# Seven parts in a row: the order of a fast matrix product's parts and downs, and the split of one conversion

## The reference

```python
# 1: attention with top-32 scores, 2 batches x 8 heads x 576 x 64
scores = scale * q @ k.T;  keep scores >= 32nd largest;  x = softmax(scores) @ v
# 2: x is 1152 x 512
x = ((x @ w_a) * (x @ w_b)) @ w_out                     # 512 -> 1536 -> 512
# 3: four experts, w1 512 x 1024, w2 1024 x 512
p = domain_probs / (domain_probs.sum(-1) + 1e-9)
for e in range(4):
    out += p[:, e:e+1] * (np.maximum(x @ w1[e], 0) @ w2[e])
```

## Time and profile before

| | |
|---|---|
| median of 3 runs | 832.29 us (831.46 to 832.82) |
| the profiled execution | 832.34 us |
| its span, first to last instruction | 830.5 us |
| TensorE busy (matmuls) | 783.9 us, 94% |
| VectorE, ScalarE, GpSimd busy | 571.9, 436.8, 362.1 us |
| mean granted clock of TensorE | 0.977 |

### The profile page before, as it was taken

How to read it: one execution, slowest core, us unless ns; L and a number is a source line. 1 busy time by engine, 2 the same in 40 slices (tenths; PEclk the granted TensorE clock), 3 DMA queues, 4 the chain that set the end, 5 groups by cost and what they waited for, 6 DMA issues and landing times.

```text
span 830.5 us, 14209 instructions
## 1 busy us (share of the span) xinstructions
PE 783.9 (94%) x5141; PEld 687.2 (83%) x5141; DVE 571.9 (69%) x1144; ACT 436.8 (53%) x848; POOL 362.1 (44%) x325
## 2 busy tenths in 40 slices
PE   5469899999999999999999899999999999999998
PEld 3247778888888888888897798889988898989987
DVE  6999998989999999998444543573345634483333
ACT  6687768777777777776555422342133422343221
POOL 1868773545444444445335421463035521364010
PEclk9677999999999999999999999999999999999999
DMA  9450775466545484445578002310031002120101
GB/s 240 127 154 1 242 251 175 153 189 199 178 152 175 150 281 144 160 146 184 184 244 253 0 8 69 93 36 1 26 102 52 26 1 77 56 72 1 51 1 63
DMA packets 80709, 97.93 MB, mean 118 GB/s; under 512 B 32896, under 2 KB 60032, under 8 KB 80640
## 3 DMA queue, kind: packets, MB, share of 16 engines
q1 hardware_dynamic: 79584, 96.77, 36.9%
q10 hardware_dynamic: 1056, 0.26, 0.1%
HBM read 86.00 MB, written 11.01 MB: 117 GB/s over the span
## 4 chain that ended last, share of the span: by engine, by line
PE 82%; DVE 7%; ACT 4%; issue 3%; POOL 2%; DMA 1%; ACTq 0%; SPq 0%; POOLq 0%; DVEq 0%
PE ps L795 23%; PE ps L727 21%; PE ps L634 15%; PE ps L619 8%; PE ps L547 4%; PE ps L583 4%; PE ps L560 3%; DVE m L1132 2%; DVE work L1138 2%; PE ps L592 2%; DVE work L1126 1%; POOL p_sb L1355 1%; DMA wo<-wo_d 1%; DVE m L1122 1%; ACT s_sb L878 1%
## 5 line engine op out<-in xcount | busy, mean ns | idle before, releaser
L1132 DVE MAX8 m<-work 128x8 f32<-128x576 f32 x216 | 152.7, 751 | 0.0
L727 PE MATMUL ps<-x_hi,w_hi 128*128 128x256 f32 (+1 forms) x448 | 133.1, 297 | 5.2 <-ACT p_sb L983 4.8
L795 PE MATMUL ps<-w_lo,h_hi 128*128 128x512 f32 x288 | 113.7, 395 | 0.0
L795 PE MATMUL ps<-w_hi,h_hi 128*128 128x512 f32 x288 | 113.4, 394 | 0.0
L795 PE MATMUL ps<-w_hi,h_lo 128*128 128x512 f32 x288 | 113.1, 393 | 0.0
L1355 POOL TENSOR_TENSOR p_sb<-s_sb,p_sb 128x576 f32<-128x576 f32 x72 | 101.9, 1432 | 20.5 <-ACT p_sb L884 19.9
L1416 POOL TENSOR_TENSOR u_sb<-u_sb,p_sb 128x256 f32<-128x256 f32 (+1 forms) x32 | 30.6, 956 | 174.2 <-DVE u_sb L1255 174.2
L1138 DVE MATCH_REPLACE8 work<-m,work 128x576 f32<-128x576 f32 x144 | 106.3, 747 | 0.0
L727 PEld LDWEIGHTS ps<-x_hi,w_hi 128*128 128x128 f32 x448 | 84.9, 190 | 14.6 <-ACT p_sb L983 5.7
L995 ACT ACTIVATE h_hi<-u_sb 128x256 fp32r<-128x256 f32 (+1 forms) x64 | 28.5, 445 | 106.8 <-POOL u_sb L1416 81.0
L727 PE MATMUL ps<-x_raw_lo,w_hi 128*128 128x256 f32 (+1 forms) x256 | 76.2, 298 | 0.0
(11 more groups left out here) (124 smaller groups left out, 2027.9 us busy)
## 6 DMA issues: line engine op xcount, KB each, us to landing
wo<-wo_d SPq DMA_DIRECT2D x96, 512.0 KB, 4.8
w_raw<-moe_w_in SPq DMA_DIRECT2D x32, 256.0 KB, 3.3
w_raw<-moe_w_in SPq DMA_DIRECT2D x16, 512.0 KB, 4.8
wo_d<-wo SPq DMA_DIRECT2D x12, 512.0 KB, 4.5
w_raw<-moe_w_a_in SPq DMA_DIRECT2D x4, 768.0 KB, 5.4
w_raw<-moe_w_b_in SPq DMA_DIRECT2D x4, 768.0 KB, 5.3
wo_raw<-moe_w_out_in SPq DMA_DIRECT2D x12, 256.0 KB, 3.3
x_d<-x_out_sb SPq DMA_DIRECT2D x9, 256.0 KB, 3.0
```

The lines of the kernel that those rows point to most:

```text
L727: mm = nc.tensor.matmul(ps[:, bank, 0:NH[g]], w, x, start=first and c == n == 0, stop=last and c == HK - 1 and n == 2, skip_group_check=True)
L795: mm = nc.tensor.matmul(ps[:, DOWN_BANKS[j], 0:DM], h[:, f, tok], w[:, f, :], start=m == f == n == 0, stop=m == FM - 1 and f == 1 and n == 2)
L1132: nc.vector.max(m8[:, par, i, 8 * r:8 * r + 8], work[:, i, :]).then_inc(ve_top, 1)
```

## The change

TensorE: step k runs P1, P5, P6, P2, P3, P7, then all downs of step k-1 (tile by tile, both halves of a tile together), then P4. In step 0 the last `send` stands where the downs stand.

SyncE: `load_x2` is split into its two halves and each waits for the stores it needs; for the second group the first half is issued early. The loads of w1's quarter 2 are issued ahead of the last reloads of w_out.

ScalarE and VectorE: the preparation of the second token group is cut into pieces that stand between the copies of steps 2 and 3. In step 0 `w2_high`, `y_out` and `x2_out` stand later. The buffers u3 and c21 are placed elsewhere.

```diff
-            def load_x2(g):
-                sp.wait_ge(st_x2, 16 * (TILES[0] if g == 0 else NT))
-                for j in range(2):
...
+            def load_x2(g, j):
+                first = TOK[g] + j * NH[g]
+                sp.wait_ge(st_x2, 16 * -(-(first + NH[g]) // P))
...
-            for n in range(LAST + 2):
+            for n in range(LAST + 1):
                 slot_loads(n)
             sp.wait_ge(pe_a, NP)
             sp.wait_ge(pe_b, NP)
             load_w1(0, 2)
+            slot_loads(LAST + 1)
             load_w2(0, 1)
             load_w1(0, 3)
+            load_x2(1, 0)
             load_w2(0, 2)
             slot_loads(LAST + 3)
+            load_x2(1, 1)
             sp.wait_ge(pe_w, FC * NP)
             load_w2(0, 3)
-            load_x2(1)
...
-            def downs(k, first, last):
-                tiles = TILES[step(k)[1]]
-                for i in range(first, min(last, 2 * tiles)):
-                    down(k, i // tiles, i % tiles)
+            def downs(k):
+                for j in range(TILES[step(k)[1]]):
+                    for f in range(2):
+                        down(k, f, j)
+
+            def seven(k, between):
+                p1(k)
+                p5(k)
+                p6(k)
+                p2(k)
+                p3(k)
+                p7(k)
+                between(k - 1)
+                p4(k)
 
             send(NP - 2)
             h_transpose(NP - 1)
-            p1(0)
-            p5(0)
-            p6(0)
-            send(NP - 1)
-            p2(0)
-            p3(0)
-            p7(0)
+            seven(0, lambda k: send(NP - 1))
             y_transpose(NT - 1)
-            p4(0)
             for k in range(1, STEPS):
-                few = step(k - 1)[1] == 0
-                a, b, c, d, f = (1, 2, 3, 5, 7) if few else (1, 3, 5, 7, 9)
-                p1(k)
-                downs(k - 1, 0, a)
-                p5(k)
-                downs(k - 1, a, b)
-                p6(k)
-                downs(k - 1, b, c)
-                p2(k)
-                p3(k)
-                downs(k - 1, c, d)
-                p7(k)
-                downs(k - 1, d, f)
-                p4(k)
-                downs(k - 1, f, 2 * TILES[1])
+                seven(k, downs)
...
@@ step_copies on ScalarE
                 p5_out(k)
                 if q1 is not None:
                     w1_high_raws(q1)
+                if k == FM - 2:
+                    x2_high_piece(1, 0)
+                if k == FM - 1:
+                    x2_high_piece(1, 2)
                 act.wait_ge(pe_p2, k + 1)
...
                     w1_high_sums(q1)
+                if k == FM - 2:
+                    x2_high_piece(1, 1)
+                if k == FM - 1:
+                    x2_high_piece(1, 3)
...
@@ step 0 on ScalarE
             p5_out(0)
-            w2_high(0)
-            y_out(NT - 1)
...
             hidden_high(0, 0, 1, ac_h12)
-            x2_out(NT - 1)
+            w2_high(0)
+            y_out(NT - 1)
...
             hidden_high(0, 1, 0, ac_h21)
+            x2_out(NT - 1)
...
@@ the steps on VectorE
                 if k and w1_prepared(k) is not None:
                     w1_sums(w1_prepared(k))
+                if k == FM - 2:
+                    x2_sums(1, True)
                 u2(k)
...
                 hidden_low(k, 0, 1, ac_h12, ve_l12)
+                if k == FM - 2:
+                    x2_sums(1, False)
+                if k == FM - 1:
+                    x2_low_piece(1, 2)
...
-                if k == 2:
-                    x2_sums(1)
-                    for i in range(len(X2_PIECES)):
-                        x2_low_piece(1, i)
+                if k == FM - 2:
+                    x2_low_piece(1, 0)
+                    x2_low_piece(1, 1)
+                if k == FM - 1:
+                    x2_low_piece(1, 3)
```

More of the change, by code:

```diff
@@ L87, in build @@
         x2_out_sb = sb("x2_out_sb", [P, DK, P])
+        inv_at = top[0]
         inv_b = sb("inv_b", [P, DM])
@@ L182, in build @@
         late_at += 2 * W2B
-        u3_sb = at("u3_sb", [P, NH[1]], F32, late_at)
-        c21_sb = at("c21_sb", [P, NH[1]], F32, late_at + TEMP)
-        assert late_at - 2 * W2B <= w_end and late_at + 2 * TEMP <= ring_at
+        u3_sb = at("u3_sb", [P, NH[1]], F32, inv_at)
+        c21_sb = at("c21_sb", [P, NH[1]], F32, late_at)
+        assert late_at - 2 * W2B <= w_end and late_at + TEMP <= ring_at
         def w1_whole(m, i):
@@ L412, in keep_x2 @@
                 sp.dma_start(dst, x2_out_sb[:]).then_inc(st_x2, 16)
-            def load_x2(g):
-                sp.wait_ge(st_x2, 16 * (TILES[0] if g == 0 else NT))
-                for j in range(2):
[L417 to L420, removed]
+            def load_x2(g, j):
+                first = TOK[g] + j * NH[g]
+                sp.wait_ge(st_x2, 16 * -(-(first + NH[g]) // P))
+                src = x2_d.rearrange("(c p) n -> p c n", p=P)[:, :, first:first + NH[g]]
+                dst = x2_parts[g][0][:, 2 * j:2 * j + 2, :, :].rearrange("p h c n -> p (h c) n")
+                sp.dma_start(dst, src).then_inc(ld_x2[g], 16)
             def slot_loads(n):
@@ L455, in slot_loads @@
                         load_w1(0, m)
-                    load_x2(0)
-            for n in range(LAST + 2):
+                    load_x2(0, 0)
+                    load_x2(0, 1)
+            for n in range(LAST + 1):
                 slot_loads(n)
@@ L963, in x2_high_piece @@
             def x2_high_piece(g, i):
-                if i == 0:
-                    act.wait_ge(ve_t[g], 4)
+                act.wait_ge(ld_x2[g], 32)
+                if i:
+                    act.wait_ge(ve_t[g], 3 if i == 1 else 4)
                 raw, sums, hi = x2_parts[g][0:3]
@@ L1106, in _ @@
                 step_copies(k)
-                if k == 2:
-                    for i in range(len(X2_PIECES)):
-                        x2_high_piece(1, i)
         @block.vector
@@ L1203, in w1_sums, with x2_sums @@
                 add(part[6], part[1], part[5], ALU.subtract, ve_s, 4 * q + 2)
-            def x2_sums(g):
-                dve.wait_ge(ld_x2[g], 32)
+            def x2_sums(g, first):
                 part = [x2_whole(g, i) for i in range(7)]
[L1208 to L1211, removed]
+                if first:
+                    dve.wait_ge(ld_x2[g], 32)
+                    add(part[5], part[2], part[0], ALU.subtract, ve_t[g])
+                    add(part[6], part[3], part[5], ALU.subtract, ve_t[g], 1)
+                else:
+                    add(part[2], part[3], part[2], ALU.subtract, ve_t[g])
+                    add(part[4], part[1], part[6], ALU.subtract, ve_t[g], 2)
             def x2_low_piece(g, i):
                 dve.wait_ge(ac_x2[g], i + 1)
+                dve.wait_ge(ve_t[g], 4)
                 raw, sums, hi, raw_lo, sum_lo = x2_parts[g]
@@ L1293, in _ @@
                         nc.vector.tensor_tensor(pr_n[:, :, e], pr_raw[:, :, e], pr_inv[:], ALU.mult).then_inc(ve_pr, 1)
-                    x2_sums(0)
+                    x2_sums(0, True)
+                    x2_sums(0, False)
             for i in range(2):
```

## The result

The changed kernel takes 852.05 us (median of 6, 848.76 to 856.15) against 832.32 us before (831.46 to 833.05): ratio 1.024, 95% interval 1.0205 to 1.0274. The forecast was 850.0 us. The profiled execution took 848.76 us with a span of 847.0, 16.5 us over the span of before. It is the fastest of the six: what follows explains 16.5 us, the medians lie 19.7 us apart, and no profile shows the 3.3 us between.

The account below looks back on a forecast made before the run. The last stage's second product was taken as bound by TensorE's own stream. Steps 0 to 4 cost 9.65 less 5.7 us (+3.9), six later steps +13.8: 832.3 + 17.7 = 850.0 us, likeliest case 846 to 855, overall 839 to 858.

Parts of the forecast that it names:

- The six later steps: Steps 8, 9, 16, 17, 24, 25: P7 waits for u2 behind a held addition; 2.15 or 2.45 us each, +13.8 us.
- Rest: Other waits and steps (P4 for u3, P6 for c21, P3, loads, final downs): put at nothing.
- Step 0: Wait for the w_out chunk and restarts go, y_out lies bare before the transposes: net -0.5 us, bounds -0.9 and +1.2.
- Step 1: P2 waits for ScalarE's copy of P1 without downs ahead: TensorE idles 3.0 instead of 0.75 us, +2.1 us.
- Step 2: Two second-group additions stand ahead of u2, the later one held: stall 2.4 + 0.1 us; 0.8 unheld, 3.1 both held.
- Steps 3 and 4: Low pieces delay u2 in step 3 (3.05 + 0.1 us) and P1 in step 4 (2.3 + 0.1), less 5.7 lost before.
- The row at 478.21: w2_low(3) begins within the last two low pieces, which took 2.22 us unheld while GpSimd took 3.07; speaks for 2 us less.
- the unheld bound: Step 3: stall of 1.1 us if VectorE's low pieces are not held behind GpSimd's w2_low.
- VectorE isn't held: Rival: additions and pieces beside w2_low run unheld; +1.1 us, 833.4 us, no change that shows; chance 0.08.
- the clock falls as well: Rival: clock falls after the new waits, 1.6 us each; 853.2 us with two falls, 866 with all ten; chance 0.16.
- the pieces go unheld: Rival: pieces unheld in steps 2 and 3, additions held; 3.5 us less, 846.5 us; chance 0.15.
- The slack that I gave P3: In w2_high steps P5's copy is done at about c + 2.4, P3 ready at 2.7: 0.3 us spare, no cost.

Follow-up runs that it names:

- pool_fill: Changed kernel with w2_low waiting for w1_sums, plus idle matmuls into an unused PSUM bank before P2 (step 1), P7 (step 3), P1 (step 4): 836.62 us, ratio 1.0057.
- old_fixed: Changed kernel with TensorE's old order, u2 ahead of w1_sums and the second group's additions, its low pieces moved: 830.88 us, ratio 0.9993 to the kernel before.

## Why the prediction was right, point by point

*The six later steps.* Forecast 13.8 us, measured 15.5, of which 1.6 are the one fall of the clock in step 8. The waits were 2.05 and 2.35 by forecast, 2.00 and 2.21 in the trace; with the restarts I had 2.15 and 2.45 a step, and the five steps without a fall took 2.15, 2.19 and three times 2.47 more. The mechanism is shown four ways: the old order put back, u2 moved, GpSimd moved, cover given back. The reading that carried it is that VectorE's and ScalarE's chain from c21 hangs on nothing that TensorE's new order changes, so its length could be copied from the earlier trace rows.

*Rest.* I put it at nothing, on the ground that a part or a down takes the same whichever kind went before. The 22 other steps from step 4 on took 1.3 us less: small, but there in 21 of the 22.

*Step 0.* Forecast -0.5, measured -1.1. I had y_transpose ahead of P4 in the new order, as before. The diff has P4 first, and y_out lies under it: an order read wrongly, 0.6 us.

*Step 1.* Forecast +2.1, measured +3.2. The wait was 3.1 us where I had 3.0. The clock fell in it (0.60), a cost that I kept for a rival; the wait of P3 that I had isn't there.

*Step 2.* Forecast +2.5, measured 0.0. I took one addition as held on the ground that the two requests came at the same time. In the profile after, VectorE was ahead by 0.07 us. *pool_fill*, with 2.25 us, shows that the mechanism was right; that the fall of the clock in step 1 had hidden it in the changed kernel is what its rows point to.

*Steps 3 and 4.* Forecast 3.15 + 2.4 - 5.7 = -0.15, measured +1.2. The waits were 3.14 and 2.16 us, where I had 3.05 and 2.3. The difference is the clock in step 3 (0.57), again the rival's term. GpSimd, which asked ahead of the second piece, went first, as the Trainium skill's rule in "SBUF — State Buffer", section "Who interferes with whom", has it; the two pieces took 5.05 us instead of 2.89. The row at 478.21 that spoke for the unheld bound can be read after all, in a view that begins behind the third piece:

```profile
478.22 0.82 DVE L1219 TENSOR_TENSOR x_sum_lo<-x_sum,x_hi 128x640 fp32r<-128x640 f32 x1
```

The two were given at the same time to 0.01 us, and VectorE went first. In step 3 of the changed kernel they lie 0.48 us apart.

So the terms that I put at 3.9 and 13.8 came out at 3.3 and, with the rest, 14.2. The wait of step 2 that failed to come (-2.5), step 0 (-0.6) and the rest (-1.3) worked against three falls of the clock (1.6 us in that of step 8): that the sum came so close is in part luck. *The rivals:* that VectorE isn't held is refuted by each trace; that the clock falls as well was right for three of the ten waits, and its price of 1.6 us is what step 8 shows; that the pieces go unheld came true in step 2 and not in step 3.

Left open: where the spread between the runs of the changed kernel (7.4 us against 1.6) comes from. The clock can be only a part of it. One fall of 3.4 us lowers the mean granted clock by 0.002; the executions of 848.76, 852.1 and 855.75 us had 0.972, 0.972 and 0.970. The slack that I gave P3 in the w2_high steps (0.3 us) held in the changed kernel, but wore out to waits of 0.24 us when u2 went ahead; steps 9, 17 and 25 then took 11.12 us each, against 10.63 before.

## What to carry to other kernels

When a kernel is bound by one engine's stream, regrouping that stream wins next to nothing in itself (here less than 0.1 us a step); it moves cover. Measure, for each wait it leaves bare, the other engines' chain from its own trigger in the old trace, and compare that with the cover that stays. An operation that is the first reader's on its queue (here u2) belongs ahead of work that only has to be done sometime, but look at what that work then meets: here it fell under GpSimd's subtractions, and with the old order the wait moved from P7 to P4.

## What the runs showed of the hardware

A VectorE subtraction or addition with both inputs in SBUF that is given after a GpSimd subtraction or addition has begun is held until that one is done. It ends 0.28 us behind it with 256 columns (2.59 instead of 0.42 us), 0.68 with 640 (2.88 instead of 0.82, *pool_fill*), 1.35 with 1280 (3.53 instead of 1.49, *old_fixed*). In the fourteen traces, from 430 us on, each one that began 0.05 us or more behind GpSimd's recorded start was held, and each one that began ahead of it, or 0.01 us behind, ran at its own pace. GpSimd's row is then the longer one: 3.03 us instead of 2.4 to 2.6 beside the 0.82 us of VectorE. No operation of VectorE with an input in PSUM (u2, c12, accumulations) was held in them: beside a running GpSimd the longest took 0.43 us with 256 columns and 0.75 with 512.

The clock fell after a wait of 2.00 us at 543.99 (0.57 in the 3.4 us behind it, 15.69 us for the step) and did not after the same wait at 644.56 (14.07 us for the same step of the next expert). In the fourteen traces the clock fell in or behind each of the fourteen waits of 2.9 to 5.0 us, behind 5 of the 19 waits of 2.0 to 2.3 us that began at the full clock, and behind none under 1.9 us. A wait of 2 us costs its length or 1.6 us more, and which of them it is changes from wait to wait.
